# A greedy router and the first expert layer as one program: each expert placed when its phase of the search ends, the next phase's steps beside its blocks

## The reference

```
h = gated scan of x                                  # layer 1
logits = h @ moe_w_gate                              # N x 8
for idx in argsort(-logits.flatten()):               # layer 2: greedy routing
    tok, e = idx // 8, idx % 8
    if assigned[tok] < 0 and counts[e] < N // 8:     # cap 2528 rows for each expert
        assigned[tok] = e; counts[e] += 1
for e in range(8):
    y[assigned == e] = relu(h[assigned == e] @ moe_w1[e]) @ moe_w2[e]   # 256 -> 1024 -> 256
out = top-1 mixture of 8 experts on y, weighted by its gate             # layer 3
```

## Time and profile before

| what | us |
|---|---|
| median of 3 runs (lowest, highest) | 2631.3 (2627.9, 2635.2) |
| profiled execution, its own time | 2632.9 |
| its span | 2631.1 |
| scan stage | 0 to 211.8 |
| routing, and the first block's rows | 211.8 to 596.0 |
| 40 blocks of layer 2 | 596.0 to 1596.6 |
| change of stage | 1596.6 to 1628.3 |
| layer 3 | 1628.3 to 2631.1 |
| busy: PE, DVE, ACT, POOL | 2264.8, 1480.4, 748.4, 1016.5 |

### The profile page before, as it was taken

The page is one execution under the profiler, slowest core; times in us unless marked ns, Lnnn a source line. Parts: engine busy times, 40 slices in busy tenths (PEclk is TensorE's granted clock), DMA queues, the critical chain, the costliest instruction groups (busy, mean ns, idle before and its releaser), DMA issues. The chain is left out here.

```text
span 2631.1 us, 53310 instructions
## 1 busy us (share of the span) xinstructions
PE 2264.8 (86%) x16585; PEld 2086.6 (79%) x16586; DVE 1480.4 (56%) x4148; ACT 748.4 (28%) x1836; POOL 1016.5 (39%) x1199
## 2 busy tenths in 40 slices
PE   6883333449999999999999995999999999999997
PEld 5772222328888888888888884999999999999997
DVE  6886777786565657565657564433334343333333
ACT  3440000042222222222222221333333333333332
POOL 3442000024444444344444534444535543535333
PEclk9995555589999999999999997999999999999999
DMA  7992000011112111111111112212212121211111
GB/s 246 339 329 80 0 0 0 0 40 48 57 55 64 56 56 58 54 64 56 56 60 56 60 44 60 80 39 78 75 42 74 46 76 44 73 45 47 38 48 36
DMA packets 86281, 182.99 MB, mean 70 GB/s; under 512 B 14334, under 2 KB 50945, under 8 KB 86082
## 3 DMA queue, kind: packets, MB, share of 16 engines
q0 software_dynamic: 31872, 85.58, 10.4%
q1 hardware_dynamic: 33474, 76.05, 8.3%
q10 hardware_dynamic: 20864, 20.71, 2.5%
HBM read 119.99 MB, written 64.13 MB: 70 GB/s over the span
## 5 line engine op out<-in xcount | busy, mean ns | idle before, releaser
L1652 DVE SCALAR_TENSOR_TENSOR m_hl<-m_hP,m_hh 128x256 fp32r<-128x256 f32 x664 | 281.7, 424 | 516.5 <-ACT m_hh L1611 516.5
L1611 ACT ACTIVATE m_hh<-m_hP 128x256 fp32r<-128x256 f32 x664 | 254.6, 383 | 500.2 <-PE m_hP L1562 499.9
L1277 DVE SCALAR_TENSOR_TENSOR m_hl<-m_hP,m_hh 128x512 fp32r<-128x512 f32 x320 | 220.8, 690 | 260.0 <-ACT m_hh L1236 256.8
L1236 ACT ACTIVATE m_hh<-m_hP 128x512 fp32r<-128x512 f32 x320 | 191.6, 601 | 611.8 <-PE m_hP L1176 611.5
L1129 POOL DMA_INDIRECT y_rows<-m_rows,m_dest x164 | 165.7, 1010 | 407.8 <-issue 400.2
L1327 DVE SCALAR_TENSOR_TENSOR m_product<-w_raw,m_wgb 128x256 f32<-128x256 f32 x512 | 215.9, 467 | 2.5 <-issue 2.5
L1500 POOL DMA_INDIRECT m_xg<-y_rows,m_idx x170 | 167.7, 987 | 101.2 <-POOL m_idx L1496 70.3
L742 PE MATMUL wide_ps<-above,choice 128*64 128x128 bf16 x500 | 73.7, 314 | 147.7 <-DVE above L867 147.7
L1117 POOL DMA_INDIRECT m_xg<-h_rows,m_idx x164 | 160.2, 977 | 73.3 <-issue 39.8
L1511 POOL DMA_INDIRECT out_dram<-m_rows,m_dest x166 | 168.1, 1013 | 51.3 <-issue 50.0
L742 PEld LDWEIGHTS wide_ps<-above,choice 128*64 128x64 bf16 x500 | 50.0, 162 | 167.7 <-DVE above L867 167.7
(11 more groups left out here) (315 smaller groups left out, 5911.4 us busy)
## 6 DMA issues: line engine op xcount, KB each, us to landing
w_raw<-in_moe_w_dram SPq DMA_DIRECT2D x32, 1024.0 KB, 5.0
f_in<-in_f_logit_dram SPq DMA_DIRECT2D x39, 512.0 KB, 5.2
x_in<-in_x_dram SPq DMA_DIRECT2D x39, 512.0 KB, 6.5
h_rows<-rows ACTq DMA_DIRECT2D x39, 512.0 KB, 5.9
m_xg<-y_rows,m_idx POOLq DMA_INDIRECT x170
out_dram<-m_rows,m_dest POOLq DMA_INDIRECT x166, 2.5
m_xg<-h_rows,m_idx POOLq DMA_INDIRECT x164, 2.8
y_rows<-m_rows,m_dest POOLq DMA_INDIRECT x164, 2.5
```

Of the source, the lines that this page charges most:

```text
L1236: act.activation(hh[f % 2][:], hP[f % 2][:], ACT.Relu).then_inc(hh_ready, 1)
L1277: dve.scalar_tensor_tensor(out=hl[f % 2][:], in0=hP[f % 2][:], scalar=0.0, in1=hh[f % 2][:].bitcast(F32), op0=ALU.max, op1=ALU.subtract).t ...
L1611: act.activation(hh[f % AHEAD][:], hP[f % AHEAD], ACT.Relu).then_inc(hh_ready, 1)
L1652: dve.scalar_tensor_tensor(out=hl[f % AHEAD][:], in0=hP[f % AHEAD], scalar=0.0, in1=hh[f % AHEAD][:].bitcast(F32), op0=ALU.max, op1=ALU.su ...
```

## The change

`route_greedy`, `place*` and `experts_greedy` become one function, `route_and_experts`, without barriers between. Phase 0 and the placing of the first full expert come first. Then 40 blocks run, written out without loops. Beside the blocks of the expert in place o, each engine takes steps of phase o+1 out of a table by slot n = 8j+f (block j of 5, step f of 8), through three functions called `beside`, one for each of PE, ACT and DVE. The full experts are computed in the order in which they fill up, so SP reads the number of the weights from a register. In detail:

- A round counts with two halves instead of four pieces, and one fp32 matmul of 128 columns gives all experts' sums on all partitions (`allP`) instead of two small ones.
- Placing is by expert: `members`, `slots`, then 10 groups of 16 columns (`hits`), 16 matmuls each with 40 moving columns (`products`), `finish`.
- The second gate's columns come from PE: 16 transposes of w2 and 16 fp32 matmuls of 8 columns an expert. DVE's 64 products go.
- Weights are split by ACT (high) and DVE (low), no longer by POOL.
- `rows`, `xh`, `xl` have two buffers; `tP` is one PSUM bank; ACT copies all four tiles at a block's end.

In the diff, the `beside` shown is PE's (it runs behind down(n)), `hand` is ACT's, and the last loop is DVE's.

```diff
-        route_greedy(nc, c, moe_w1, moe_w2, moe2_w_gate)
-        experts_greedy(nc, c, h_rows, moe_w1, moe_w2, moe2_w1, moe2_w2, y_rows)
+        route_and_experts(nc, c, h_rows, moe_w1, moe_w2, moe2_w_gate, moe2_w1, moe2_w2, y_rows)
...
+FIRST_ROUND = 6
+TRY = FIRST_ROUND + 4 * TRIED
+MEMBERS = TRY + 3
+LAST_MEMBERS = 6
+CASTS = 28
+GATED = 35
+LOWS = {33: (0, 1), 34: (2,), 35: (3, 4), 36: (5, 6), 37: (7,), 38: (8,)}
...
+            def count_half(k, r, half):
+                n = k * ROUNDS + r
+                pe.wait_ge(above_ready, 2 * n + half + 1)
+                for q in range(half * groups // 2, (half + 1) * groups // 2):
+                    mm = pe.matmul(cP, columns(q), above[:, :, q * Q:(q + 1) * Q], start=(q == 0), stop=(q == groups - 1))
+                if half == 1:
+                    mm.then_inc(counted, 1)
...
+            def products(k, g):
+                pe.wait_ge(hits_ready, k * GROUPS + g + 1)
+                pe.wait_ge(row_part, k * GROUPS + g + 1)
+                for j in range(GROUP):
+                    mm = pe.matmul(foundP, hit_place[:, g % 2, j // 2, :, j % 2], hit_row[:, g % 2, j // 2, :, :, j % 2],
...
+            def beside(o, n):
+                k = o + 1
+                if k < PH:
+                    if FIRST_ROUND <= n < FIRST_ROUND + 4 * TRIED:
+                        r, part = divmod(n - FIRST_ROUND, 4)
+                        if part < 2:
+                            count_half(k, r, part)
+                        elif part == 2:
+                            all_counts(k, r)
+                    elif n == TRY:
+                        exact_if_over(k)
+                if k < E:
+                    at = MEMBERS if k < PH else LAST_MEMBERS
+                    if n == at:
+                        member_base(k)
+                    elif at + 3 <= n < at + 3 + GROUPS:
+                        products(k, n - at - 3)
+                    elif n == GATED or n == GATED + 1:
+                        through_gate(k, 2 * (n - GATED))
+                        through_gate(k, 2 * (n - GATED) + 1)
...
+            def hand(i):
+                act.wait_ge(rows_free, i + 1)
+                act.wait_ge(h_used, FC * (i + 1) + 2)
+                for k in range(TPC):
+                    ins = act.copy(rows[i % 2][:, k, :], yP[:, k, 0:WIDE])
+                ins.then_inc(rows_ready, 1)
...
+            for o in range(E):
+                for j in range(BPE):
+                    i = BPE * o + j
+                    for f in range(FC):
+                        low(i, f)
+                        if f == 0:
+                            lessen(i)
...
+                        elif f >= FC - DH:
+                            low_half(i + 1, f - FC + DH)
+                        beside(o, FC * j + f)
```

More of the change, by code:

```diff
@@ L514, in place_products @@
[L514 to L534, removed]
@@ L537, in place_parts @@
[L537 to L551, removed]
@@ L554, in place_rows @@
[L554 to L592, removed]
@@ L1132, in scatter_before @@
-                pool.wait_ge(scattered, 16 * TPC * (i + 1))
+                                            rows[(i - 1) % 2][:, k, 0:ROW].bitcast(I32), None,
+                                            bounds_check=E * N - 1, oob_is_err=False).then_inc(scattered, 16)
+            pool.wait_ge(ends_ready, 2)
+            pool.partition_all_reduce(endg[:], ends[:], P, bass.bass_isa.ReduceOp.max).then_inc(ends_all, 1)
+            gather(0)
+            for i in range(BLOCKS1):
+                if i > 0:
+                    pool.wait_ge(scattered, 16 * TPC * i)
@@ new lines, in all_counts, with count_mask @@
+            def all_counts(k, r):
+                pe.wait_ge(part_ready, k * ROUNDS + r + 1)
+                pe.matmul(allP.rearrange("p e t -> p (e t)"), c.ones[0:E * Q, :], spread[:].rearrange("m e t -> m (e t)"),
+                          start=True, stop=True).then_inc(summed, 1)
+            def count_mask(n, mask):
+                pe.wait_ge(mask_ready, n + 1)
+                for q in range(groups):
+                    mm = pe.matmul(qP, columns(q), mask[:, q * Q:(q + 1) * Q], start=(q == 0), stop=(q == groups - 1))
+                mm.then_inc(mask_counted, 1)
@@ new lines, in sum_mask, with exact_if_over @@
+            def sum_mask(n):
+                pe.wait_ge(mask_row_ready, n + 1)
+                pe.matmul(nP, c.ones[0:E * Q, :], mask_row[:], start=True, stop=True).then_inc(mask_summed, 1)
+            def exact_if_over(k):
+                pe.wait_ge(over_ready, k + 1)
+                alone(pe, passed)
+                over_now = pe.value_load(over[0:1, 0:1], min_val=0, max_val=1)
+                with pe.If(over_now > 0):
+                    for r in range(TRIED, ROUNDS):
+                        count_half(k, r, 0)
+                        count_half(k, r, 1)
+                        all_counts(k, r)
+                    count_mask(2 * k, sure)
+                    sum_mask(2 * k)
+                    pe.wait_ge(own_edge_ready, k + 1)
+                    pe.matmul(oP, c.tri[:], own_edge[:], start=True, stop=True).then_inc(before, 1)
+                    count_mask(2 * k + 1, taken)
+                    sum_mask(2 * k + 1)
+                with pe.If(over_now < 1):
+                    for sem_of_round in (counted, summed):
+                        pe.sem_inc(sem_of_round, ROUNDS - TRIED)
+                    pe.sem_inc(before, 1)
+                    pe.sem_inc(mask_counted, 2)
+                    pe.sem_inc(mask_summed, 2)
@@ L1210, in compute @@
+                bring_half(i + 1, 1)
                 down(i, b, FC - 2)
+                beside(o, FC * j + FC - 2)
                 down(i, b, FC - 1)
+                beside(o, FC * j + FC - 1)
             pe.sem_inc(h_used, 2)
+            for r in range(TRIED):
+                count_half(0, r, 0)
+                count_half(0, r, 1)
+                all_counts(0, r)
+            exact_if_over(0)
+            member_base(0)
+            for g in range(GROUPS):
+                products(0, g)
@@ L1337, in _ @@
+            try_all(0)
+            exact_if_over(0)
+            settle()
+            pick(0)
+            members(0)
+            slots(0)
+            for g in range(GROUPS):
+                hits(0, g)
+            finish(0)
+            for n in range(SPLITS):
+                split_low(0, n)
             st.do(dve.tensor_copy(tri_b[:], c.tri[:]))
@@ L1390, in _ @@
             last = BLOCKS1
-            st.at(setup + last * HAND)
             lessen(last)
```

1020 lines of the change are left out of this document (522 added, 498 removed).

## The result

The changed kernel takes 2485.6 us (median of 4 runs, 2484.3 to 2488.4), beside 2629.6 for the kernel before on the same chip: a ratio of 0.945 (95% interval 0.944 to 0.947), 144 us less.

A forecast was written before the change was run, and what follows sets the result against it. PE's queue bounds the block stage, a DVE-PE chain the routing. Routing -297 us and blocks +203 (1204 instead of 1000.6) give -94 on 2632.9, 2539, so 2538 as median; range 2505 to 2600.

The forecast's parts named there:

- Term 1: Routing stretch before the blocks: shrinks to a prologue of 87 us against 384.2, -297 us (283 to 305).
- Term 2: PE's work put beside the blocks (placing, counts, sums, transposes, gate matmuls, bases, insertions): +153 us (130 to 260).
- about a cycle for a weight column: PE's small matmuls: about 55 ns each with 64 weight columns at half clock; 65 taken for 128 at full clock.
- The lower bound of 59 us: Low end for placing's 1120 matmuls on PE, forecast at 73 us (59 to 179).
- Term 3: PE's wait for the register and branch in each phase: +21 us for five, +54 for the exact search.
- Term 4: DVE's order: low parts late in an expert's first block, 1.4 us for each of 7 experts, +10 us.
- up to 1.5: DVE's other work in a hits slot, in us, beside 0.74 and 1.75, making 4.0.
- even: Hits slots: DVE's 4.0 us against PE's 2.86 + 1.1 of products.
- Term 5: Block ends: ACT's four copies cost 0.25 us a block, +10, and 2 for the clock's start; the scatter's wait goes.
- The block start at half clock: Rival: PE's wait for ACT's copies drops the clock, 3.5 us a block instead of 0.25, +130, 2668 us; chance 0.07.
- All is cheaper: Rival: 53 ns placing matmuls, DVE never late, no clock drop at branches, prologue at full clock: 2502 us; chance 0.10.

The follow-up runs named there:

- experiment 4: Changed kernel with one buffer of rows, with POOL's weight splits back, and with both: 2528.8, 2509.7 and 2541.9 us (ratios 0.959, 0.952, 0.965).

## Why the prediction was right and wrong

The block stage by its terms. Measured sizes are differences of blocks in PE's timeline, each from up(0) to up(0): a block with nothing beside it is 24.11 us, one with eight placing groups 28.1, with four half counts and two sums 28.9, with the turns of w2 and the gate's products alone 29.1, with the exact search 76.3 where its like has 26.2, of which 1.0 is a branch. The last row but one is what the others leave.

| term | forecast | measured |
|---|---|---|
| bare blocks and block ends | 954 + 10 | 40 x 24.11 = 964 |
| placing, 70 groups | 73 + 7 | 70 x 0.5 = 35 |
| counts and sums, 18 rounds | 25 + 5 | 6 x 6/4 x 4.8 = 43 |
| transposes and gate matmuls | 36 + 4 | 7 x 5.0 = 35 |
| branches without exact search | 21 | 5 x 1.0 = 5 |
| exact search | 54 | 51 |
| late low parts in first blocks | 10 | 5 |
| bases, first matmuls at half clock, unexplained | 5 | 7 |
| sum | 1204 | 1145 |

- **Term 1 was right**, in the sum: 88.6 us forecast as 87, the first up at 300.4 in 298 +- 8. Its steps held as a sum; I didn't test them one by one.
- **The step that failed is in Term 2**, "about a cycle for a weight column": sized from the earlier trace rows, a load of 64 columns, the only small one I had looked at. It made the placing 45 us too dear, three quarters of the error: 26 ns a matmul where I had 65. The counting, 13 too cheap, is only in part its doing: with 128 weight columns 8 us of it go, and the rest is what an insertion and a sum add to the up or down behind them. The doubled placing and the wider counts show both signs. The lower bound of 59 us, from the same row, was no bound at all, and so the range ended too high.
- **Term 3 was mis-sized**: 4.2 us a branch where 1.0 shows. I let the down hide `try_all` and counted the trip in full behind it; the down also hides half of the trip, and behind the stop of 1.0 us the granted clock stayed at 1.00. The run with the later branch takes the last us away. The exact search was right within 3.
- **Term 4**: the first block's lateness was half of what I had, and a hits step on DVE takes 2.2 us from one low part to the next (722.41 to 724.62 in the rows below), not 4.0. The large comparison was priced rightly, 1.22 for 1.15; it is the other work, "up to 1.5", that is less in most steps: from nothing to 1.3. With the most of it a step takes 3.5 (718.94 to 722.41), where PE's takes 2.86 + 0.5. So "even" held only there, and elsewhere there was room.

```profile
718.94 0.68 DVE L1268 SCALAR_TENSOR_TENSOR m_hl<-m_hP,m_hh 128x512 fp32r<-128x512 f32 x1
...
722.41 0.68 DVE L1268 SCALAR_TENSOR_TENSOR m_hl<-m_hP,m_hh 128x512 fp32r<-128x512 f32 x1
723.01 0.32 DVE L1237 TENSOR_TENSOR m_hit_tile<-iota,m_slot_b 128x320 bf16<-128x320 bf16 x1
723.24 1.22 DVE L1239 TENSOR_TENSOR m_hit_place<-iota,m_slot_b 128x2048 bf16<-128x2048 bf16 x1
724.38 0.32 DVE L1241 TENSOR_TENSOR m_hit_row<-m_hit_tile,m_grid_col 128x320 bf16<-128x320 bf16 x1
724.62 0.69 DVE L1268 SCALAR_TENSOR_TENSOR m_hl<-m_hP,m_hh 128x512 fp32r<-128x512 f32 x1
```

- **Term 5** gave the right time by luck. The 10 us for block ends were in the kernel before already: its block without a wait is 24.16 us from up(0) to up(0), not the 23.86 that I added up from parts, and after it is 24.11. The waits did go, but the runs don't bear out the reason given, POOL's splits and the single buffer: with both put back the old waits stay away, and what held DVE at an expert's start is open (experiment 4). That in the changed kernel a scatter lands late beside a weight load wasn't in the forecast either.
- **The rivals.** The block start at half clock didn't come: the granted clock is 0.98. "All is cheaper" was the right direction with a chance of 0.10, and even its 2502 was too high, since its 53 ns came from the same row.

## What to carry to other kernels

Before pricing a small matmul, list the weight loads by form and compare those with 128 columns to those with fewer; padding a load to 128 bf16 columns can be a gain. A bound from one row bounds only what is of its kind: two rows of different shape would have shown that this one ran the wrong way. For work beside a full engine, the room in each step decides, not the sum: what a step adds to an engine that idles there costs next to nothing (131 us of products, 4 us), and a second buffer is worth what the transfers beside it make it worth.

## What I had not expected of the hardware

- A bf16 matmul with 128 weight columns and 40 moving ones takes 26 ns at full clock; with 64 weight columns 39 to 44.
- DVE's comparison of 320 bf16 elements goes from 0.30 to 1.98 us beside POOL's split, more than six times.
- A scatter's landing goes from 1.3 to 2.1 us after the last issue to 3.4 to 6.6 beside a load of weights (2 MB, 220 GB/s in all over 12 us).
- In the traces, four of twelve branches in the two kernels with doubled placing, and none in the others, stopped PE for 3.5 to 4 us.
- In the kernel before, DVE began the first low part of an expert 1.8 to 2.1 us after its input was ready, and the profile doesn't say why.
